# Mixing two pairs of heads in a row on TensorE at every second pair, in place of one pair at each pair

## The reference

```
scores = q @ k.T / sqrt(D) + bias        # bias: slope of the head times the distance
a = exp(scores - max);  a = a / (sum(a) + 1e-9)
x = a @ v                                # per head; "mixing" is this product
h = x @ w_in;  solu = h * softmax(h);  ln = norm(solu) * g_ln;  y = ln @ w_out
yn = y / rms(y) * rms_g
out = (silu(yn @ w_gate) * (yn @ w_val)) @ w_down
```

## Time and profile before

| | us |
|---|---|
| median of 3 runs | 586.93 |
| lowest and highest run | 586.19, 586.95 |
| the profiled execution, its own time | 585.97 |
| its span, first to last instruction | 584.2 |
| granted TensorE clock, mean | 0.977 |
| busy: PE, DVE, ACT, POOL | 539.8, 453.6, 283.5, 143.8 |

### The profile page before, as it was taken

How to read it: one execution, slowest core, us unless ns; L and a number is a source line. 1 busy time by engine, 2 the same in 40 slices (tenths; PEclk the granted TensorE clock), 3 DMA queues, 4 the chain that set the end, 5 groups by cost and what they waited for, 6 DMA issues and landing times.

```text
span 584.2 us, 10632 instructions
## 1 busy us (share of the span) xinstructions
PE 539.8 (92%) x3481; PEld 462.2 (79%) x3481; DVE 453.6 (78%) x949; ACT 283.5 (49%) x625; POOL 143.8 (25%) x259
## 2 busy tenths in 40 slices
PE   1796999999998999995979799999999999999997
PEld 1565777777776777774879799999999999999996
DVE  4769878877986878885797977787697787787765
ACT  3668566776677687743755422332242242242221
POOL 4541222123233343334624503003003003000000
PEclk9996899999999999996999899999999999999999
DMA  8656343443354253021412021001102102100013
GB/s 216 196 149 182 109 122 83 127 126 109 89 169 137 77 160 106 4 89 54 143 38 73 1 70 40 1 8 66 37 1 72 36 0 72 36 0 1 6 68 144
DMA packets 24833, 46.99 MB, mean 80 GB/s; under 512 B 2908, under 2 KB 9064, under 8 KB 24792
## 3 DMA queue, kind: packets, MB, share of 16 engines
q1 hardware_dynamic: 24480, 46.48, 26.9%
q10 hardware_dynamic: 312, 0.01, 0.0%
HBM read 40.18 MB, written 6.29 MB: 80 GB/s over the span
## 4 chain that ended last, share of the span: by engine, by line
PE 72%; DVE 17%; issue 4%; POOL 3%; ACT 2%; DMA 1%; DVEq 0%; ACTq 0%; SPq 0%; POOLq 0%
PE hidden L459 9%; PE hidden L460 9%; PE hidden L461 9%; PE turned L459 3%; PE turned L461 3%; PE turned L460 3%; PE mixed L1554 3%; PE scores_a L460 3%; PE scores_a L459 3%; PE scores_b L459 3%; PE scores_b L461 3%; PE scores_b L460 3%; PE scores_a L461 3%; PE turned L1539 2%; PE scores_a L1526 2%
## 5 line engine op out<-in xcount | busy, mean ns | idle before, releaser
L890 ACT ACTIVATE acts<-gate 128x512 fp32r<-128x512 f32 x36 | 22.8, 634 | 130.0 <-DVE gate L1343 120.6
L794 ACT ACTIVATE probs_t<-turned 116x512 f32<-116x512 f32 x48 | 28.7, 597 | 58.5 <-PE turned L1539 58.5
L459 PE MATMUL hidden<-down_hi,acts 128*128 128x512 f32 x144 | 56.5, 393 | 0.0
L460 PE MATMUL hidden<-down_lo,acts 128*128 128x512 f32 x144 | 56.5, 392 | 0.0
L461 PE MATMUL hidden<-down_hi,acts 128*128 128x512 f32 x144 | 56.3, 391 | 0.0
L1358 DVE TENSOR_TENSOR out_acc<-hidden,out_acc 128x512 f32<-128x512 f32 x60 | 41.4, 690 | 11.8 <-PE hidden L461 10.3
L784 ACT ACTIVATE probs<-logits,neg_max 128x232 f32<-128x232 f32 x96 | 45.6, 480 | 6.0 <-DVE neg_max L1185 6.0
L459 PE MATMUL hidden<-in_hi,xt_hi 128*128 128x512 f32 x96 | 44.3, 461 | 1.1 <-DVE xt_lo L1208 0.9
L459 PE MATMUL turned<-yt_hi,w_hi 128*128 128x256 f32 x144 | 41.3, 287 | 3.5 <-DVE yt_lo L1290 3.5
L733 POOL TENSOR_TENSOR sums<-w_raw 128x512 f32<-128x512 f32 x5 | 6.9, 1383 | 142.9 <-DMA w_raw<-w_val 142.9
L461 PE MATMUL turned<-yt_hi,w_lo 128*128 128x256 f32 x144 | 41.1, 286 | 0.0
(11 more groups left out here) (185 smaller groups left out, 1663.3 us busy)
## 6 DMA issues: line engine op xcount, KB each, us to landing
qk_raw<-qk_pairs SPq DMA_DIRECT2D x96, 180.0 KB, 3.2
v_in<-v_windows SPq DMA_DIRECT2D x12, 448.0 KB
y_spill<-y_out SPq DMA_DIRECT2D x12, 256.0 KB, 4.2
y_in<-y_spill SPq DMA_DIRECT2D x6, 512.0 KB, 4.7
w_raw<-w_gate SPq DMA_DIRECT2D x6, 512.0 KB, 3.7
w_raw<-w_val SPq DMA_DIRECT2D x6, 512.0 KB, 4.7
down_raw<-w_down SPq DMA_DIRECT2D x6, 512.0 KB, 3.7
out<-out_acc SPq DMA_DIRECT2D x12, 256.0 KB, 2.0
```

The source lines that it names most:

```text
L459: pe.matmul(acc, hi, other_hi, start=first, stop=False)
L460: pe.matmul(acc, hi, other_lo, start=False, stop=False)
L794: nc.scalar.activation(probs_t[:, p % 2], turned[0:HALF, :], ACT.Copy).then_inc(probs_t_ready, 1)
L890: nc.scalar.activation(act_hi[:, half].rearrange("p f n -> p (f n)"), gate[:, half], ACT.Copy).then_inc(act_rounded, 1)
```

## The change

In slots 0 and 2 nothing is mixed any more. At the end of slots 1 and 3 two pairs are mixed in a row, first the pair of the slot before, then the slot's own. Tile -1 (L1682 to L1687 of before) has a branch of its own and stays as it was.

```diff
                     if known(t) and p < 3 and (t, p) in turn_at:
                         turn_y(turn_at[t, p])
-                    mix_pair(a, 1 - even, p)
+                    if p % 2:
+                        mix_pair(a, 1 - even, p - 1)
+                        mix_pair(a, 1 - even, p)
```

## The result

| | before | after |
|---|---|---|
| median of 13 runs each, us | 586.90 | 588.27 |
| lowest, highest | 585.73, 588.77 | 587.68, 590.01 |
| profiled execution, span | 585.97, 584.2 | 588.27, 586.2 |
| granted clock, mean | 0.977 | 0.980 |

What follows compares the result with a forecast made beforehand. VectorE bounds from slot 3's `take_logits` to xt_lo, TensorE from slot 1 to slot 3. Terms 0.44 + 0.33 + 2 x (-0.06) + 3 x 0.15 - 0.24 + 0 + 2 x 0.25 = +1.36 us: 588.3, range 586.5 to 590.0.

Steps and rivals of the forecast that it cites:

- Rival B: The delay is absorbed in slot 3's `take_logits` or the first two tiles: -0.3 to +0.5 us, time 587.0; chance 0.18.
- What bounds the kernel: In loop tiles VectorE bounds from slot 3's `take_logits` to xt_lo, then TensorE from slot 1 to slot 3.
- Rival A: Changes of shape are on the path: all 22 x 0.34 = 7.5 us come off, time 579.4; chance 0.06.
- nothing comes of it: Slot 0, loop tiles: pair 0 leaving makes TensorE 0.78 us earlier, but hidden in slot 1 still waits for xt_lo.
- the forecast 0.6: Sign in the changed profile: TensorE idle some 0.6 us before hidden in slot 1, by xt_lo.
- Tiles 2 to 10: -0.06 us each in 2, 4; +0.15 in 3, 5, 6; -0.24 in 7; 0 in 8; +0.25 in 9, 10.
- the guess that part of the 0.64 us wait would stay: Tiles 2 and 4, slot 3's `take_logits`: part of the wait is register-target handling that follows h_neg; -0.06 us each.
- tile 7: Pair's 0.44 vanishes in `turn_ln`'s 0.89 us wait, leaving 0.5; VectorE's 0.29 wait in slot 3 mostly goes: -0.24 us.
- Tile 0: Slot 0's gain is lost waiting for GpSimd's in_lo; joint mixing makes slot 2 late: +0.44 us, between 0 and 0.44.
- Tile 1: Adds 0.44 us in slot 1, hardly covered; a rising clock gives back up to 0.22: +0.33, between +0.2 and +0.44.
- Moved as a whole: What follows tile 10 hangs on VectorE's and GpSimd's chain and only shifts; the second layer keeps its length.
- Rival C: TensorE's clock rises later in tiles 0 and 1: 591.3 us, half of it 589.8; sign lower clock in 60 to 70; chance 0.14.

Runs made afterwards that it cites:

- the second set of runs: The changed kernel once more, no edit, against the kernel before: 589.13 us against 586.79, ratio 1.0038.
- slot 3 front: Against before: pairs 1 and 2 mixed in a row behind the scores of slot 3, pair 3 ending slot 3, pair 0 ending slot 0; 583.10 us, ratio 0.9945.
- half 2+3: Against before: only pair 2 mixed together with pair 3 at the end of slot 3, pairs 0 and 1 alone as before; 585.44 us, ratio 0.9975.
- pair 0 mixed twice: Changed kernel with pair 0 mixed once more at the end of slot 0; 589.26 us beside the changed kernel's 589.13, ratio to before 1.0038.
- a third place: Pairs 1 and 2 mixed behind the scores of slot 3, pair 3 ending slot 3, pair 0 ending slot 0; 583.10 us, ratio to before 0.9945.

## Why the prediction was right, point by point

**The time.** 588.3 was forecast, 588.27 measured. The agreement to a few hundredths is luck: the parts are off by more, in both directions, executions of one kernel differ by 3 us, and the second set of runs gave +2.3 us. Rival B, a delay that is absorbed, is out by both intervals.

**What bounds the kernel.** Right. TensorE and VectorE take turns; the 7.5 us of TensorE's time did not come off. They were not worth quite nothing either: the emptier slot 0 pays for pair 2 in slot 3 (below). Tried from both sides: the half that puts mixing between hidden of slot 1 and slot 3 costs 0.42 to 0.44 in each of tiles 2 to 6, the half that takes it out of there gains.

**Rival A, the changes of shape.** The price of a change of shape was read rightly (joining saves the step out and in, see the 1.02 for two pairs against 0.59 for one; and scores with no mixing ahead of them have a first step of 0.11, 107.29 to 107.40 in slot 3 front, and not 0.21). As a forecast of the time it failed, since 22 fewer of them gave a slower kernel. The Trainium skill, "TensorEngine Tiling (Array Packing)", section "Tiling Modes", says that changing the tiling mode drains TensorE. The trace agrees, with these 0.34 us; whether the kernel gets them back depends on the slot in which they lie.

**Slot 0, "nothing comes of it".** Right in what it gives, xt_lo still decides when hidden starts, but the step forgot that pair 2 in slot 3 makes TensorE 0.44 later there. Had pair 0 stayed, hidden would have come late, as the half 2+3 and pair 0 mixed twice show. Idle before hidden in slot 1 is then not the forecast 0.6. Timeline of TensorE, tile 3, after:

```profile
99.32 0.40 PE L461 MATMUL y_acc<-out_hi,ln_lo 128*128 128x512 f32 x1
99.75 0.37 PE L1526 MATMUL scores_a<-qk_hi 128*128 128x232 f32 x1
99.95 0.27 PE L1527 MATMUL scores_a<-k_lo,qk_hi 128*128 128x232 f32 x1
...
100.46 0.49 PE L459 MATMUL hidden<-in_hi,xt_hi 128*128 128x512 f32 x1
```

The scores start 0.43 behind the product where 0.23 is its step, so 0.2 of waiting (for `split_qk`), and hidden another 0.17: together 0.37. The same slip made two expectations too good, that of half 2+3 and that of pair 0 mixed twice.

**Tiles 2 to 10.** Forecast +0.59 in sum, measured +0.45 and +0.42. Tiles 2 and 4 to the hundredth (-0.06 forecast, -0.05 to -0.07), with the guess that part of the 0.64 us wait would stay: h_neg to `take_logits` is now 0.37 (130.37 to 130.74), against 0.26 in tile 3. Tile 3 lost 0.24 to 0.27 and not 0.15: `take_logits` of slot 3 is 0.18 later against hidden of slot 1, and from there to the next slot 1 it takes 9.35 to 9.38 in place of 9.30. In tiles 2 and 4 this last stretch is unchanged, as the prediction took it to be. In tile 7 the wait of `turn_ln` fell from 0.89 to 0.45, as forecast, and the gain was 0.38, not 0.24, since the wait for scores went with its handling:

```profile
186.61 0.63 PE L1598 MATMUL turned_x<-ident,gated 128*128 128x128 f32 x4 [0.45 <-ACT staging L840]
...
191.68 0.22 DVE L1216 TENSOR_SCALAR h_neg<-h_max 128x1 f32<-128x1 f32 x1
191.81 0.39 DVE L1185 CUSTOM_DVE_ANT_0 logits<-scores_a,bias 128x232 f32<-128x232 f32 x1
```

**Tile 0.** Mis-sized, in two parts of opposite sign: 0.62, not 0.44. The point at which slot 0's gain is lost, in_lo, was named; that the gain would itself make in_lo later, by VectorE running into GpSimd, was missed, and is 0.38. The pair was put at its full 0.44, and is 0.24, since it fills 0.20 in which the scores waited for `split_qk`. The expectation for the change in tiles 0 and 1 split the 0.62 as 0.44 for the pair and 0.18 for GpSimd, and had both parts wrong.

**Tile 1.** Forecast +0.33; the profiles of after show -0.08 and -0.56, those of before 0 and +0.39, and 0.63, 0.23, 0.12, 1.12 in other kernels that join 0+1 there, -0.08, -0.64 and -0.69 in those that don't. The mechanism that was named, a clock that rises at some time and gives back what it catches, is larger than the term. The mean of these is no estimate. By the medians, the change in tiles 0 and 1 alone costs 1.3 us, where 0.77 was forecast.

**Behind tile 10.** "Moved as a whole" is not what a profile shows: from slot 1 of tile 11 to the first product of the second layer the second profile of before gained 1.0 us on the first, and those of after gained 0.4 and 0.6. The clock falls at different times there too. Rival C, that the change itself brings more low clock, has nothing to show for it: in 60 to 70, the stretch that was named as its sign, the granted clock is 0.91 and 0.95 in the profiles of after, 0.88 and 0.84 in those of before, and the mean clock is 0.98 in both profiles of after and in the second of before, 0.977 in the first.

**What stays open.** The steady tiles (0.42 to 0.45) and tile 0 (0.62) make 1.04 to 1.07 of the measured 1.4 to 2.3 us, and of tile 0's part the 0.38 by GpSimd is one that the kernel before may lose as well. The rest lies in tile 1 or behind tile 10, where executions of one kernel differ by more than that. From slot 1 of tile 11 to the end the two profiles of after take 0.7 and 0.5 us more than the second of before. Whether the change moves the odds there can't be told from one or two profiles per kernel.

## What to carry to other kernels

An engine that is busy 92% of the span may still not be the one to relieve: find the stretches in which the others wait for it, and count only what lies in them. When work is batched to save a switch, the batch has to stand at one of its old places, so ask for each which wait ends last there. Here two equal moves in one edit had opposite signs (-1.35 and +3.85 us), and a third place was better than both. And before two profiles are subtracted, look at the clock stretch by stretch: here 1.5 us of 2.05 came from where the clock was low in the second layer, and went away with a second profile of before.

## What the runs showed of the hardware

- A block of 116 x 64 fp32 matmuls between 128 x 128 ones costs 0.34 us beside its matmuls: 0.09 ahead, 0.15 behind, 0.10 in the first step after it. Two blocks in a row, with a satisfied semaphore wait between them, pay it once (1.02 us in place of 2 x 0.59 to the next matmul).
- The low stretches of TensorE's clock don't stand still: in 292 to 304 the same kernel had 1.00 in one execution and 0.86 in the next, and its second layer was 1.4 us longer.
- GpSimd and VectorE stall each other by whole instructions: a VectorE instruction of 0.80 us took 1.79 behind one of GpSimd's, and starting VectorE's 1.4 us earlier made GpSimd's pair 0.38 us longer. A start at 37.89 was early enough for that and one at 37.99 was not.
